# A fused convolution and two gated layers: a hand-written order of the repeated chunk on every engine

## The reference

```python
# 1: causal convolution with 7 softmax weights per head
out = np.einsum('hk,bskhg->bshg', w, x_unf)
# 2: gated layer, 192 -> 1536 -> 192
gate = 1.0 / (1.0 + np.exp(-(x @ w_gate)))
x = (gate * (x @ w_val)) @ w_out
# 3: rational layer, 192 -> 2048 -> 192
h = x @ w_in
P = a[0] + a[1] * h + a[2] * h**2 + a[3] * h**3
Q = 1.0 + np.abs(b[0]) * np.abs(h) + np.abs(b[1]) * h**2
return (P / (Q + 1e-06)) @ w_out2
```

## Time and profile before

| | |
|---|---|
| median of 3 runs | 1366.97 us (1366.0 to 1368.45) |
| the profiled execution | 1366.47 us, of which the span from first to last instruction is 1364.7 |
| TensorE, VectorE, ScalarE, GpSimd busy | 1285.5, 1245.7, 1122.5, 637.5 us |
| mean granted clock of TensorE | 0.988 |
| DMA | 23.66 MB, mean 17 GB/s |

### The profile page before, as it was taken

The page is one execution under the profiler, slowest core; times in us unless marked ns, Lnnn a source line. Parts: engine busy times, 40 slices in busy tenths (PEclk is TensorE's granted clock), DMA queues, the critical chain, the costliest instruction groups (busy, mean ns, idle before and its releaser), DMA issues.

```text
span 1364.7 us, 16882 instructions
## 1 busy us (share of the span) xinstructions
PE 1285.5 (94%) x5440; PEld 1026.4 (75%) x5440; DVE 1245.7 (91%) x1201; ACT 1122.5 (82%) x1278; POOL 637.5 (47%) x337
## 2 busy tenths in 40 slices
PE   4889999999999999999999999999999999999876
PEld 3767787777778777777777778777777877778654
DVE  7759999999999999999999999999999999998998
ACT  5468889888888888889888888888888888888774
POOL 1423545454454553554554454554454455455532
PEclk9989999999999999999999999999999999999978
DMA  7100000010100001000010100001010000000000
GB/s 202 38 0 20 1 12 21 1 31 0 31 0 11 20 0 31 0 19 12 4 27 0 31 0 12 19 0 31 0 31 0 8 23 0 19 0 12 1 12 12
DMA packets 15960, 23.66 MB, mean 17 GB/s; under 512 B 2240, under 2 KB 10048, under 8 KB 15936
## 3 DMA queue, kind: packets, MB, share of 16 engines
q1 hardware_dynamic: 14160, 21.30, 5.6%
q10 hardware_dynamic: 1776, 2.06, 0.6%
HBM read 13.13 MB, written 6.29 MB: 14 GB/s over the span
## 4 chain that ended last, share of the span: by engine, by line
PE 55%; DVE 22%; issue 9%; POOL 8%; ACT 5%; DVEq 0%; DMA 0%; POOLq 0%; SPq 0%; ACTq 0%
POOL frac_low L733 8%; PE up_ps L306 7%; PE up_ps L307 6%; PE up_ps L308 6%; PE up_ps L310 6%; PE up_ps L309 6%; DVE denom L903 5%; PE acc_main L313 5%; DVE denom L893 5%; PE acc_main L314 4%; PE acc_tail L317 4%; PE acc_tail L315 4%; PE acc_main L316 4%; DVE frac_high L884 2%; DVE numer L874 2%
## 5 line engine op out<-in xcount | busy, mean ns | idle before, releaser
L733 POOL TENSOR_TENSOR frac_low<-denom,seed 128x1024 fp32r<-128x1024 f32 x126 | 334.3, 2653 | 626.4 <-DVE denom L903 591.8
L724 POOL TENSOR_TENSOR gated_low<-gated,gated_high 128x512 fp32r<-128x512 f32 x192 | 286.5, 1516 | 67.4 <-ACT gated_high L545 67.4
L306 PE MATMUL up_ps<-x_high,up_high 128*128 128x512 f32 x640 | 255.5, 399 | 43.5 <-DVE x_low L935 15.9
L307 PE MATMUL up_ps<-x_high,up_low 128*128 128x512 f32 x640 | 252.3, 394 | 0.0
L308 PE MATMUL up_ps<-x_low,up_high 128*128 128x512 f32 x640 | 252.3, 394 | 0.0
L310 PE MATMUL up_ps<-x_tail_low,up_tail 128*128 128x512 f32 x640 | 251.5, 393 | 0.0
L309 PE MATMUL up_ps<-x_tail_high,up_tail 128*128 128x512 f32 x640 | 251.3, 393 | 0.0
L556 ACT ACTIVATE seed<-up_ps,coef 128x1024 f32<-128x1024 f32 x128 | 143.0, 1117 | 85.5 <-POOL frac_low L733 46.8
L866 DVE TENSOR_TENSOR numer<-up_ps,numer 128x1024 f32<-128x1024 f32 x128 | 156.3, 1221 | 52.9 <-ACT numer L565 32.3
L306 PEld LDWEIGHTS up_ps<-x_high,up_high 128*128 128x128 f32 x640 | 121.3, 189 | 81.3 <-DVE denom L856 17.4
L565 ACT ACTIVATE numer<-up_ps,coef 128x1024 f32<-128x1024 f32 x128 | 153.9, 1202 | 25.0 <-DVE denom L903 18.4
(11 more groups left out here) (88 smaller groups left out, 2273.7 us busy)
## 6 DMA issues: line engine op xcount, KB each, us to landing
x_raw<-x_chunks SPq DMA_DIRECT2D x16, 393.0 KB, 3.1
out_chunks<-out_main SPq DMA_DIRECT2D x16, 256.0 KB, 2.1
tail_twice<-conv SPq DMA_DIRECT2D x60, 64.0 KB, 2.0
out_chunks<-tail_part SPq DMA_DIRECT2D x16, 128.0 KB, 2.3
numer<-w_out SPq DMA_DIRECT2D x1, 1536.0 KB, 7.2
seed<-w_out ACTq DMA_DIRECT2D x1, 1152.0 KB, 11.0
denom<-w_in SPq DMA_DIRECT2D x2, 512.0 KB, 5.1
denom<-w_gate SPq DMA_DIRECT2D x1, 576.0 KB, 5.3
```

Source lines behind the costliest of these rows:

```text
L306: nc.tensor.matmul(acc, up_high[:, cols], x["high"][:], start=True, stop=False)
L307: nc.tensor.matmul(acc, up_low[:, cols], x["high"][:], start=False, stop=False)
L724: nc.gpsimd.tensor_tensor(gated_low[:, b], gated[:, b], gated_high[:, b], ALU.subtract).then_inc(gated_low_done, 1)
L733: nc.gpsimd.tensor_tensor(ring(frac_low, j, 2, LOW_RING), ring(denom, j), ring(seed, j), ALU.mult).then_inc(frac_low_done, 1)
```

## The change

Three things. The function that wrote one sequence for each window is replaced by `chunk(i)`, in which each quarter's steps stand in an order of their own, on TensorE, ScalarE, GpSimd and VectorE. The ramp is written out by hand (on each engine in the order that it had before), chunk 2 is the first to use `chunk(i)`, and the loop still covers 3 to 14. The body of the loop starts at another place: the first pair of h of quarter 0 is issued at the end of the chunk ahead. Second, the semaphore `x1_low` becomes `x1_main_low` and `x1_tail_low`, and `out_copied` becomes `out_main_copied` and `out_tail_copied`; TensorE's `down_gated` for tile 0 waits for the sum of x1's tail and no longer for its low part. Third, helpers test themselves whether their chunk exists, and the weight helpers are split in two; the instructions they issue are the same. All operations, their shapes and operands are as before.

On VectorE each `rest`, whose end lets GpSimd make the low part, stands ahead of operations of which most read PSUM (`quadratic`, `cubic`, `gate`, `sum_x1_tail`).

The diff, cut to its core (the ramp, the guards and the drain are left out; in the drain only the steps that moved into `chunk` are gone):

```diff
+FIRST_LOOPED = 2
...
-        x1_low = sem("x1_low")
+        x1_main_low, x1_tail_low = sem("x1_main_low"), sem("x1_tail_low")
...
-        out_copied, out_tail_summed = sem("out_copied"), sem("out_tail_summed")
+        out_main_copied, out_tail_copied = sem("out_main_copied"), sem("out_tail_copied")
+        out_tail_summed = sem("out_tail_summed")
...
-        def periods(eng, period):
-            for i in range(3):
-                period(i)
-            with eng.Fori(3, chunks - 1) as i:
-                period(i)
-            period(chunks - 1)
+        def chunk_loop(eng, chunk):
+            chunk(FIRST_LOOPED)
+            with eng.Fori(FIRST_LOOPED + 1, chunks - 1) as i:
+                chunk(i)
+            chunk(chunks - 1)
...
+            def store(n):
+                if isinstance(n, int) and n == chunks - 1:
+                    sp.wait_ge(last_out_copied, 1)
+                else:
+                    sp.wait_ge(out_main_copied, n + 1)
+                sp.dma_start(out_chunks[n, 0:P, :], out_main[:]).then_inc(out_main_sent, 16)
+                sp.wait_ge(out_tail_summed, n + 1)
+                sp.dma_start(out_chunks[n, P:d_model, :], tail_part[0:tail]).then_inc(out_tail_sent, 16)
+
+            def chunk(i):
+                if is_chunk(i + 1):
                     load_x(i + 1)
-                if is_chunk(i - 2):
-                    if isinstance(i, int) and i == chunks + 1:
-                        sp.wait_ge(last_out_copied, 1)
-                    else:
-                        sp.wait_ge(out_copied, 2 * (i - 1))
-                    sp.dma_start(out_chunks[i - 2, 0:P, :], out_main[:]).then_inc(out_main_sent, 16)
-                    sp.wait_ge(out_tail_summed, i - 1)
-                    sp.dma_start(out_chunks[i - 2, P:d_model, :], tail_part[0:tail]).then_inc(out_tail_sent, 16)
+                store(i - 2)
                 if is_chunk(i + 1):
                     double_tail(i + 1)
 
-            periods(sp, period)
-            period(chunks)
-            period(chunks + 1)
+            double_tail(1)
+            load_x(2)
+            double_tail(2)
+            chunk_loop(sp, chunk)
+            store(chunks - 2)
+            store(chunks - 1)
...
-                        pe.wait_ge(x1_low, 2 * i)
+                        pe.wait_ge(x1_main_low, i)
+                        pe.wait_ge(x1_tail_low, i)
...
-                        after(pe, out_copied, 2 * (i - 1))
+                        after(pe, out_main_copied, i - 1)
...
-                        after(pe, x1_low, 2 * i)
+                        after(pe, x1_main_low, i)
+                        after(pe, x1_tail_summed, 2 * i)
...
+            def chunk(i):
+                down_fraction(i - 1, 2, 1)
+                down_gated(i - 1, 3, 0)
+                down_gated(i - 1, 3, 1)
+                down_gated(i - 1, 3, 2)
+                up_gate(i, 0, 0)
+                up_gate(i, 0, 1)
+                up_gate(i, 0, 2)
+                up_val(i, 0, 0)
+                up_val(i, 0, 1)
+                up_val(i, 0, 2)
+                up_h(i, 1, 0)
+                up_h(i, 1, 1)
+                down_fraction(i - 1, 3, 0)
+                down_fraction(i - 1, 3, 1)
+                down_gated(i, 0, 0)
+                up_gate(i, 1, 0)
+                up_gate(i, 1, 1)
+                down_gated(i, 0, 1)
+                up_gate(i, 1, 2)
+                up_val(i, 1, 0)
+                up_val(i, 1, 1)
+                up_val(i, 1, 2)
+                up_h(i, 2, 0)
+                down_gated(i, 0, 2)
+                up_h(i, 2, 1)
+                down_fraction(i, 0, 0)
+                down_fraction(i, 0, 1)
+                down_gated(i, 1, 0)
+                down_gated(i, 1, 1)
+                up_gate(i, 2, 0)
+                up_gate(i, 2, 1)
+                up_gate(i, 2, 2)
+                up_val(i, 2, 0)
+                up_val(i, 2, 1)
+                up_val(i, 2, 2)
+                up_h(i, 3, 0)
+                up_h(i, 3, 1)
+                down_gated(i, 1, 2)
+                down_fraction(i, 1, 0)
+                down_gated(i, 2, 0)
+                down_gated(i, 2, 1)
+                up_gate(i, 3, 0)
+                down_gated(i, 2, 2)
+                up_gate(i, 3, 1)
+                up_gate(i, 3, 2)
+                up_val(i, 3, 0)
+                up_val(i, 3, 1)
+                up_val(i, 3, 2)
+                up_h(i + 1, 0, 0)
+                down_fraction(i, 1, 1)
+                up_h(i + 1, 0, 1)
+                down_fraction(i, 2, 0)
+
+            chunk_loop(pe, chunk)
...
+            def chunk(i):
+                sigmoid(i - 1, 3, 2)
+                log_table()
+                log(i - 1, 3, 1)
+                exp(i - 1, 3, 0)
+                round_gated(i - 1, 3, 0)
+                exp(i - 1, 3, 1)
+                round_gated(i - 1, 3, 1)
+                round_x0_tail(i)
+                slope(i, 0, 0)
+                magnitude(i, 0, 0)
+                slope(i, 0, 1)
+                round_gated(i - 1, 3, 2)
+                magnitude(i, 0, 1)
+                round_x0_main(i)
+                square(i, 0, 0)
+                square(i, 0, 1)
+                log(i, 0, 0)
+                sigmoid(i, 0, 0)
+                copy_x1_part(i)
+                sigmoid(i, 0, 1)
+                round_x1_main(i)
+                sigmoid(i, 0, 2)
+                round_x1_tail(i)
+                log_table()
+                round_gated(i, 0, 0)
+                exp(i, 0, 0)
+                round_gated(i, 0, 1)
+                log(i, 0, 1)
+                slope(i, 1, 0)
+                magnitude(i, 1, 0)
+                slope(i, 1, 1)
+                magnitude(i, 1, 1)
+                square(i, 1, 0)
+                round_gated(i, 0, 2)
+                exp(i, 0, 1)
+                square(i, 1, 1)
+                log(i, 1, 0)
+                sigmoid(i, 1, 0)
+                sigmoid(i, 1, 1)
+                sigmoid(i, 1, 2)
+                log_table()
+                exp(i, 1, 0)
+                log(i, 1, 1)
+                magnitude(i, 2, 0)
+                slope(i, 2, 0)
+                exp(i, 1, 1)
+                slope(i, 2, 1)
+                magnitude(i, 2, 1)
+                round_gated(i, 1, 0)
+                square(i, 2, 0)
+                round_gated(i, 1, 1)
+                round_gated(i, 1, 2)
+                square(i, 2, 1)
+                copy_out_tail(i)
+                log(i, 2, 0)
+                sigmoid(i, 2, 0)
+                copy_out_main(i)
+                sigmoid(i, 2, 1)
+                sigmoid(i, 2, 2)
+                log_table()
+                log(i, 2, 1)
+                exp(i, 2, 0)
+                round_gated(i, 2, 0)
+                round_gated(i, 2, 1)
+                slope(i, 3, 0)
+                magnitude(i, 3, 0)
+                slope(i, 3, 1)
+                magnitude(i, 3, 1)
+                square(i, 3, 0)
+                round_gated(i, 2, 2)
+                log(i, 3, 0)
+                square(i, 3, 1)
+                exp(i, 2, 1)
+                sigmoid(i, 3, 0)
+                sigmoid(i, 3, 1)
+
+            chunk_loop(act, chunk)
...
+            def chunk(i):
+                split_gated(i - 1, 2, 2)
+                low_fraction(i - 1, 2, 0)
+                low_fraction(i - 1, 2, 1)
+                split_gated(i - 1, 3, 0)
+                split_gated(i - 1, 3, 1)
+                split_gated(i - 1, 3, 2)
+                split_x0_main(i)
+                low_fraction(i - 1, 3, 0)
+                low_fraction(i - 1, 3, 1)
+                split_gated(i, 0, 0)
+                split_gated(i, 0, 1)
+                split_gated(i, 0, 2)
+                low_fraction(i, 0, 0)
+                low_fraction(i, 0, 1)
+                split_gated(i, 1, 0)
+                split_gated(i, 1, 1)
+                split_gated(i, 1, 2)
+                low_fraction(i, 1, 0)
+                low_fraction(i, 1, 1)
+                split_gated(i, 2, 0)
+                split_gated(i, 2, 1)
+
+            chunk_loop(pool, chunk)
...
+            def chunk(i):
+                cubic(i, 0, 1)
+                denominator(i, 0, 0)
+                product(i - 1, 3, 0)
+                denominator(i, 0, 1)
+                rest(i - 1, 3, 0)
+                sum_x1_tail(i)
+                split_x1_main(i)
+                gate(i, 0, 0)
+                split_x1_tail(i)
+                gate(i, 0, 1)
+                product(i - 1, 3, 1)
+                gate(i, 0, 2)
+                rest(i - 1, 3, 1)
+                high_fraction(i, 0, 0)
+                conv_tap(i + 1, 0)
+                quadratic(i, 1, 0)
+                cubic(i, 1, 0)
+                quadratic(i, 1, 1)
+                denominator(i, 1, 0)
+                cubic(i, 1, 1)
+                high_fraction(i, 0, 1)
+                denominator(i, 1, 1)
+                product(i, 0, 0)
+                conv_tap(i + 1, 1)
+                rest(i, 0, 0)
```

(98 more changed lines are left out.)

532 lines of the change are left out of this document (323 added, 209 removed).

## The result

1353.4 us in the median of 4 runs (1352.8 to 1354.1) against 1367.6 before: 0.990 of it, interval 0.988 to 0.992. Faster by 1.0%, at the upper end of the range; the forecast was 1337. The profiled execution took 1354.1 us, span 1352.2.

The account below looks back on a forecast made before the run. The loop runs at TensorE's pace with VectorE close behind, the end at VectorE's. From 1366.5 us, less 37.4 of removed waits, plus 8.4 of new ones, came 1337.5 (forecast 1337), range 1326 to 1354.

Parts of the forecast that it names:

- Pace and count: TensorE's matmuls need 78.1 us of an 81.26 us chunk; three removable waits cost 2.82 per chunk, 37.4 over the run.
- x1: TensorE's wait for x1's low part, 0.65 us per chunk, goes as lead grows from 4.5 to 6.8 us; spare 0.7.
- Second fraction pair of quarter 1: Moved behind quarter 3's ups on TensorE; its low-fraction wait of 0.65 us per chunk goes, with much to spare.
- Second fraction pair of quarter 3: TensorE's low-fraction wait of 1.52 us per chunk goes, barely: low part ready at 19.0, wanted at 19.5.
- (b): GpSimd's low product of quarter 0's first pair ends inside a conv tap's slot and may push it by 0.5 us.
- New tight places: Three places with little spare in the new order, put at 0.6 us of new waits per chunk, 8.4 in all.
- (a): Quarter 2: low part of quarter 1's gated tiles ready at 41.1, wanted by down1 at 41.4.
- (c): Denominator of each quarter's first pair ends 0.4 to 1.4 us ahead of the gate tile that takes its bank.
- Ramp and drain at nothing: Ramp (chunks 0 and 1) kept in old order, drain changed only in its first few steps: no effect for both.
- Signals: Split semaphores let TensorE's down1 restart when x1's tail is summed; it isn't needed sooner, so nothing.
- Rival 1: Half comes back: the tight places each take a wait, 1.8 us per chunk in all, 1354 us; chance 0.20.
- Rival 3: Slower through the shared port: GpSimd's low products hold VectorE's operations; three full holds give 1386 us; chance 0.09.

Follow-up runs that it names:

- e2: Changed kernel with the sigmoid's table loaded by an instruction of its own ahead of quarter 0's first sigmoid on ScalarE; 1338.5 us, ratio 0.979.
- e1: Changed kernel with the copy of x1's part put ahead of quarter 0's first sigmoid on ScalarE; 1340.0 us, ratio 0.980.
- u1: Changed kernel with down_fraction(i, 1, 1) back in its old place right behind down_fraction(i, 1, 0), ahead of quarter 3's ups; 1367.6 us, ratio 1.001.
- e3: Changed kernel with VectorE's last steps before chunk 2 put in the loop's order, separating two high fractions; 1351.1 us, ratio 0.988.
- e4: Changed kernel with the edits of both e1 and e3; 1336.6 us, ratio 0.978.
- s1: Kernel before, all orders kept, with x1_low and out_copied split and down1's restart waiting for the sum of x1's tail; 1367.0 us, ratio 1.000.
- p1: Changed kernel; on VectorE the sum of the output's tail and the high fraction behind the rest of quarter 1's second pair swapped; 1354.7 us, ratio 0.991.

## Why the prediction missed

The mechanism, removed waits on TensorE with VectorE and GpSimd unchanged in their work, was right, and the sign with it. The size was a little under half of the forecast. By its steps:

- *Pace and count* (78.1 us of matmuls, 2.82 of waits, 37.4 in all): holds. e2's chunk is 78.5, the pace and about the 0.4 that I had left as spread.
- *x1*: the failed step. The chain "ends by my walk at 11.9", then "The 0.65 goes; spare 0.7". It ended at 13.2 on that scale (638.30 - 625.10, the first step of the chunk), 1.3 us late, as much as one table load takes (1.28). The chain as the prediction lists it has no load at all; that fits only if the load runs while ScalarE waits for the gate tile. It stands behind that wait, and sigmoid, copy, sums and splits stand behind it. Its own cost is 0.87 us per chunk where the prediction had none; with what went with it, 13.4 (e1) to 14.9 us (e2) of the run: nearly the whole miss of 16.4.
- *Second fraction pair of quarter 1*: the wait went. u1 shows that the move was needed, but for another pair's wait: put back in its old place, the pair itself does not wait.
- *Second fraction pair of quarter 3*: the low product behind the high fraction took 3.30 (forecast 3.4) and was in time. The conv tap of place (b) is held: 1.38 in place of 1.01, 0.37 late where I had 0.5.
- *New tight places, 0.6 per chunk*: (a) measured 0.27, (b) nothing on TensorE, (c) some 0.1 twice, 0.5 in all; once x1 is in time (e1, e2) 0.2 to 0.3. So that term was slightly too large.
- *Ramp and drain at nothing*: failed. I compared the orders of the ramp up to chunk 2 and missed that VectorE's last five steps there are neither the old order nor the loop's. That was 2.3 (e3) to 3.4 us (e4). The end was 2.4 longer in the profiled pair, and no run shows what made it so.
- *Signals*: nothing, as forecast (s1).
- Rival 1 gave 1354 by waits spread over several tight places. The time is that, the mechanism is not: one wait of 0.87 at a place that it did not name, and losses at the entry and the end. That the numbers meet is chance.
- Rival 3 happens in small: holds of 0.3 to 0.5 us at four operations of VectorE per chunk, paid from its spare time; p1 could not make it large.

The rule of the Trainium skill named in the prediction, "SBUF — State Buffer", section "Who interferes with whom", says that whichever is first has the port for its whole instruction. The holds at 598.31 and 1258.66 agree: both operations end 1.1 us behind the end of GpSimd's, nearly their whole usual length. p1's row does not, if first means the earlier start in the trace.

## What to carry to other kernels

In a schedule laid out by hand, ask of each instruction what the engine really does while it waits: one that the compiler puts in for another (a table load) waits for what that one waits for. Give it a place of its own, or put in front whatever needs no table. And after a new order for the loop, lay the entry and the exit against the loop's order step by step: in the profiled executions the entry and the end took back 4.7 of 17.4 us.

## What the runs showed of the hardware that I had not expected

- The table load of 1.28 us inserted for an activation starts only when that activation's semaphore has come: 1.72 us idle, then 1.28 of load. As an instruction of its own it starts 0.02 us after the log ends, and no second load follows.
- GpSimd's operation, listed from 601.02, did not hold a high fraction that started at 601.38, and was itself lengthened by 1.5 us; started 2.5 us ahead (595.77), GpSimd did hold a rest at 598.31, by 0.3.
- Behind a wait of 3.1 us the granted clock fell to half for most of 151.57 to 155.52 (0.57 in the mean, starts 0.43 apart in place of 0.23), and behind the 5.2 us in the drain it was 0.50. It does not follow from the one wait alone: behind the same 2.63 us in chunk 1 the changed kernel's profile has half clock for 3.4 us (from 107.7), e3's has full clock.
